# Attention scores: from two products over 128 rows per block to three products over 64 rows, two heads side by side

## The reference

```python
scores = scale * np.matmul(q, k.transpose(0, 1, 3, 2))
scores = cap * np.tanh(scores / cap)
attn = np.exp(scores - max)
attn = attn / (sum + 1e-09)
x = np.matmul(attn, v)                          # to (1792, 768)
h = np.maximum(np.maximum(x @ w1, x @ w2), x @ w3)
x = h @ w_out
silu = g * (1.0 / (1.0 + np.exp(-g)))           # g = x @ w_gate
out = (silu * (x @ w_val)) @ w_out2             # width 1536 between
```

## Time and profile before

| | |
|---|---|
| median of three runs | 1102.54 us |
| profiled execution, its own time | 1104.76 us |
| its span, first to last instruction | 1102.8 us |
| mean granted TensorE clock | 0.998 of full |
| PE busy | 1085.2 us, 98% |
| PE weight loads (PEld) busy | 980.7 us, 89% |
| DVE, ACT, POOL busy | 582.6, 475.2, 121.1 us |

### The profile page before, as it was taken

One profiled execution on the slowest core, in us unless ns is written; L12 is line 12 of the kernel. 1 busy time (PEld: TensorE's weight loads), 2 busy tenths in 40 slices (PEclk: granted clock), 3 DMA queues, 4 the chain that ended last, 5 costly groups with the idle time before them and its releaser, 6 DMA issues.

```text
span 1102.8 us, 13696 instructions
## 1 busy us (share of the span) xinstructions
PE 1085.2 (98%) x5232; PEld 980.7 (89%) x5232; DVE 582.6 (53%) x794; ACT 475.2 (43%) x601; POOL 121.1 (11%) x72
## 2 busy tenths in 40 slices
PE   6999999999999999999999999999999999999998
PEld 3669999999998999999999999999999999999998
DVE  3998777988961555557553354555664212122310
ACT  5965444444433353454452434434443322332322
POOL 0105444444340000000000000000000000000000
PEclk9999999999999999999999999999999999999999
DMA  7566763754848577577476856765555766666664
GB/s 182 121 162 219 261 211 125 265 194 144 267 148 265 180 214 210 175 213 216 171 221 224 252 177 208 220 188 197 182 172 183 234 232 208 225 210 219 218 227 134
DMA packets 98897, 222.68 MB, mean 202 GB/s; under 512 B 31249, under 2 KB 34321, under 8 KB 98833
## 3 DMA queue, kind: packets, MB, share of 16 engines
q1 hardware_dynamic: 95376, 216.31, 62.1%
q10 hardware_dynamic: 3456, 5.51, 1.3%
HBM read 192.68 MB, written 29.10 MB: 201 GB/s over the span
## 4 chain that ended last, share of the span: by engine, by line
PE 92%; ACT 3%; issue 2%; DMA 2%; SPq 0%; DVE 0%; ACTq 0%
PE moe_ps L340 78%; PE score_ps L265 6%; PE pv_ps L292 5%; PE pv_ps L297 3%; ACT prob L395 2%; DMA lo_store<-w_lo 1%; DMA qk_raw<-qk_in 1%; ACT sums L405 0%; DMA stage<-w_in 0%; ACT w_hi L386 0%; PE moe_ps L279 0%; ACT prob L398 0%; PE pv_ps L279 0%; ACT L395 0%; SPq L189 0%
## 5 line engine op out<-in xcount | busy, mean ns | idle before, releaser
L340 PE MATMUL moe_ps<-x_lo,w_hi 128*128 128x448 f32 x1008 | 369.1, 366 | 0.0
L340 PE MATMUL moe_ps<-x_hi,w_hi 128*128 128x448 f32 x1008 | 368.9, 366 | 0.0
L340 PE MATMUL moe_ps<-x_hi,w_lo 128*128 128x448 f32 x1008 | 368.5, 366 | 0.0
L386 ACT ACTIVATE w_hi<-stage 128x768 fp32r<-128x768 f32 x240 | 202.3, 843 | 341.6 <-DMA stage<-w_in 212.0
L340 PEld LDWEIGHTS moe_ps<-x_hi,w_hi 128*128 128x128 f32 x1008 | 189.7, 188 | 16.1
L340 PEld LDWEIGHTS moe_ps<-x_hi,w_lo 128*128 128x128 f32 x1008 | 189.9, 188 | 15.1
L340 PEld LDWEIGHTS moe_ps<-x_lo,w_hi 128*128 128x128 f32 x1008 | 189.9, 188 | 15.0
L340 PE MATMUL moe_ps<-gv_hi,w_hi 128*128 128x448 f32 x432 | 157.9, 365 | 0.0
L340 PE MATMUL moe_ps<-gv_lo,w_hi 128*128 128x448 f32 x432 | 157.9, 365 | 0.0
L340 PE MATMUL moe_ps<-gv_hi,w_lo 128*128 128x448 f32 x432 | 157.7, 365 | 0.0
L249 POOL TENSOR_TENSOR w_lo<-stage,w_hi 128x768 fp32r<-128x768 f32 x60 | 118.9, 1983 | 208.4 <-ACT w_hi L386 208.4
(11 more groups left out here) (50 smaller groups left out, 893.0 us busy)
## 6 DMA issues: line engine op xcount, KB each, us to landing
stage<-w_in SPq DMA_DIRECT2D x240, 384.0 KB, 4.0
w_lo<-lo_store SPq DMA_DIRECT2D x180, 384.0 KB, 3.1
lo_store<-w_lo SPq DMA_DIRECT2D x60, 384.0 KB, 3.9
qk_raw<-qk_in SPq DMA_DIRECT2D x48, 448.0 KB, 6.2
v_one<-v_in SPq DMA_DIRECT2D x48, 112.0 KB, 3.8
out<-out_sb ACTq DMA_DIRECT2D x24, 224.0 KB, 4.4
cap<-cap_in SPq DMA_DIRECT2D x1, 0.5 KB, 2.0
```

The costliest lines, as they stand in the source:

```text
L340: mm = nc.tensor.matmul(moe_ps[:, bank_of(u), 0:SEQ], w[:, u % ring, c * P:(c + 1) * P], m[:, kc, :], start=(first and c == 0 and n == 0), ...
L386: nc.scalar.activation(w_hi[:, u % R_HI, :], stage[:, u % STAGE, :], ACT.Copy).then_inc(w_hi_done, 1)
```

## The change

Each step now takes one chunk c = a % 4 of both heads. Head 0 of the pair lies on partitions 0 to 63 and head 1 on 64 to 127, for q and k alike, so that q and k are loaded once. A step has six score products over 64 rows each: for each of the three terms k_hi·q_hi, k_hi·q_lo, k_lo·q_hi one product of head 0 on the upper rows of the array and one of head 1 on the lower rows, into two different banks. The fourth term, k_lo·q_lo, is no longer made. DVE makes the high and the low part of a pair's q and k in one call of two operations, in two buffers. The sums of both heads of a pair are taken together after its last step. ACT does one tanh of a single column at the start, as soon as `cap` is loaded.

```diff
-SUMS_AT = {4: 0, 8: 1}
-PREP_AT = {3: 0, 7: 1}
+SUMS_AT = 8
+PREP_AT = 3
...
-        qk_raw = sb("qk_raw", [P, 2, 4, SEQ])
-        qk_hi = sb("qk_hi", [P, 4, SEQ], F32R)
-        q_lo = sb("q_lo", [P, 2, SEQ], F32R)
+        qk_raw = sb("qk_raw", [P, 2, 2, SEQ])
+        qk_hi = sb("qk_hi", [P, 2, 2, SEQ], F32R)
+        qk_lo = sb("qk_lo", [P, 2, 2, SEQ], F32R)
...
             def load_qk(g):
                 if g >= 2:
-                    sp.wait_ge(qk_split, 2 * (g - 1))
-                for r in range(2):
-                    sp.dma_start(qk_raw[r * HEAD_DIM:(r + 1) * HEAD_DIM, g % 2, :, :],
-                                 qk_in[g, :, :, :]).then_inc(qk_loaded[g % 2], 16)
+                    sp.wait_ge(qk_split, g - 1)
+                sp.dma_start(qk_raw[:, g % 2, :, :], qk_in[g, :, :, :]).then_inc(qk_loaded[g % 2], 16)
...
             def scores(a):
-                g, h, c = a // 4, a // 2 % 2, a % 2
-                pe.wait_ge(qk_split, 2 * g + h + 1)
+                g, c = a // 4, a % 4
+                pe.wait_ge(qk_split, g + 1)
...
-                for i in range(HALF):
-                    k0 = (HALF * c + i) * KEYS
-                    for n, q in enumerate((qk_hi[:, h, :], q_lo[:, h, :])):
-                        last = nc.tensor.matmul(score_banks(a)[0:KEYS, i, 0:SEQ],
-                                                qk_hi[:, 2 + h, k0:k0 + KEYS], q,
-                                                start=(n == 0), stop=(n == 1))
+                terms = ((qk_hi, qk_hi), (qk_hi, qk_lo), (qk_lo, qk_hi))
+                for n, (keys, queries) in enumerate(terms):
+                    for h in range(2):
+                        rows = slice(h * HEAD_DIM, (h + 1) * HEAD_DIM)
+                        last = nc.tensor.matmul(score_banks(a)[0:KEYS, h, 0:SEQ],
+                                                keys[rows, g % 2, 1, c * KEYS:(c + 1) * KEYS],
+                                                queries[rows, g % 2, 0, :],
+                                                start=(n == 0), stop=(n == 2))
...
             def take_sums(g, h):
-                act.wait_ge(value_done, 4 * g + 2 * h + 2)
+                act.wait_ge(value_done, 4 * g + 4)
...
+            act.wait_ge(cap_loaded, 16)
+            nc.scalar.activation(table_warm[:, :], cap[:, :], ACT.Tanh)
             act.wait_ge(scale_done, 2)
-            act.wait_ge(cap_loaded, 16)
             for a in range(FIRST):
                 weigh(a)
-                if a >= 2 and a % 2 == 1:
-                    take_sums((a - 2) // 4, (a - 2) // 2 % 2)
+                if a % 4 == 1 and a > 4:
+                    for h in range(2):
+                        take_sums(a // 4 - 1, h)
...
-            take_sums(PAIRS - 1, 1)
+            for h in range(2):
+                take_sums(PAIRS - 1, h)
...
-            def prepare_qk(g, h):
+            def prepare_qk(g):
                 raw = qk_raw[:, g % 2, :, :]
-                dve.wait_ge(qk_loaded[g % 2], 32 * (g // 2 + 1))
-                if g >= 1:
-                    dve.wait_ge(score_done, 4 * (g - 1) + 2 * h + 2)
-                nc.vector.tensor_copy(qk_hi[:, h::2, :], raw[:, h::2, :]).then_inc(qk_hi_done, 1)
-                dve.wait_ge(qk_hi_done, 2 * g + h + 1)
-                subtract(q_lo[:, h, :], raw[:, h, :], qk_hi[:, h, :])
-                subtract(qk_hi[low, 2 + h, :], raw[low, 2 + h, :],
-                         qk_hi[low, 2 + h, :]).then_inc(qk_split, 1)
+                dve.wait_ge(qk_loaded[g % 2], 16 * (g // 2 + 1))
+                if g >= 2:
+                    dve.wait_ge(score_done, 4 * (g - 1))
+                nc.vector.tensor_copy(qk_hi[:, g % 2, :, :], raw).then_inc(qk_hi_done, 1)
+                dve.wait_ge(qk_hi_done, g + 1)
+                subtract(qk_lo[:, g % 2, :, :], raw, qk_hi[:, g % 2, :, :]).then_inc(qk_split, 1)
...
             for g in range(PAIRS):
-                prepare_qk(g + 1, 0)
-                if g >= 1:
-                    normalise(g - 1)
-                    split_x(0, g - 1)
-                prepare_qk(g + 1, 1)
-            normalise(PAIRS - 1)
-            split_x(0, PAIRS - 1)
+                if g + 2 <= PAIRS:
+                    prepare_qk(g + 2)
+                normalise(g)
+                split_x(0, g)
```

More of the change, by code:

```diff
@@ L110, in build @@
         tanh_scale = sb("tanh_scale", [P, 1])
+        table_warm = sb("table_warm", [P, 1])
         moe_ps = ctx.enter_context(nc.psum_tensor("moe_ps", [P, BANKS, 512], F32))
@@ L158, in build @@
         sum_cols = [slice(HEAD_DIM, P), slice(0, HEAD_DIM)]
-        low = slice(HEAD_DIM, P)
         def score_banks(a):
@@ L261, in scores @@
                     pe.wait_ge(tanh_done, a - 1)
-                for i in range(HALF):
-                    k0 = (HALF * c + i) * KEYS
-                    for n, q in enumerate((qk_hi[:, h, :], q_lo[:, h, :])):
-                        last = nc.tensor.matmul(score_banks(a)[0:KEYS, i, 0:SEQ],
-                                                qk_hi[:, 2 + h, k0:k0 + KEYS], q,
-                                                start=(n == 0), stop=(n == 1))
+                terms = ((qk_hi, qk_hi), (qk_hi, qk_lo), (qk_lo, qk_hi))
[6 more added lines that the diff above has]
+                                                start=(n == 0), stop=(n == 2))
                 last.then_inc(score_done, 1)
             def values_whole(a):
-                g, h, c = a // 4, a // 2 % 2, a % 2
-                if h == 0 and c == 0:
+                g, c = a // 4, a % 4
+                if c == 0:
                     pe.wait_ge(v_loaded[g % 2], 32 * (g // 2 + 1))
@@ L276, in values_whole @@
                 pe.wait_ge(exp_done, a + 1)
[L277 to L280, removed]
+                for h in range(2):
+                    last = nc.tensor.matmul(value_banks(g)[:, h, 0:SEQ], v_one[:, g % 2, h, c, :],
+                                            prob[:, a % NP, h, :], start=(c == 0), stop=(c == CH - 1))
                 last.then_inc(value_done, 1)
             def values_split(a):
-                g, h, c = a // 4, a // 2 % 2, a % 2
-                if h == 0 and c == 0:
+                g, c = a // 4, a % 4
+                if c == 0:
                     pe.wait_ge(v_split, g - PAIRS + 1)
@@ L288, in values_split @@
                 pe.wait_ge(p_hi_done, a - FIRST + 1)
-                for i in range(HALF):
-                    j = HALF * c + i
+                for h in range(2):
                     for v in (v_hi, v_lo):
-                        nc.tensor.matmul(pv_ps[:, h, 0:SEQ], v[:, h, j, :], p_hi[:, a % NQ, i, :],
-                                         start=(j == 0 and v is v_hi), stop=False)
+                        nc.tensor.matmul(pv_ps[:, h, 0:SEQ], v[:, h, c, :], p_hi[:, a % NQ, h, :],
+                                         start=(c == 0 and v is v_hi), stop=False)
                 pe.wait_ge(p_lo_done, a - FIRST + 1)
[L295 to L298, removed]
+                for h in range(2):
+                    last = nc.tensor.matmul(pv_ps[:, h, 0:SEQ], v_hi[:, h, c, :], p_lo[:, a % NQ, h, :],
+                                            start=False, stop=(c == CH - 1))
                 last.then_inc(value_done, 1)
@@ L453, in _ @@
                     weigh(4 * g + SCORE_AT[j])
-                if g is not None and j in SUMS_AT:
-                    take_sums(g, SUMS_AT[j])
+                if g is not None and j == SUMS_AT:
+                    for h in range(2):
+                        take_sums(g, h)
             evacuate(LAST - 1)
@@ L562, in _ @@
                                     ALU.mult).then_inc(scale_done, 1)
-            for h in range(2):
-                prepare_qk(0, h)
+            prepare_qk(0)
+            prepare_qk(1)
             for g in range(PAIRS):
-                prepare_qk(g + 1, 0)
-                if g >= 1:
-                    normalise(g - 1)
-                    split_x(0, g - 1)
-                prepare_qk(g + 1, 1)
-            normalise(PAIRS - 1)
-            split_x(0, PAIRS - 1)
+                if g + 2 <= PAIRS:
+                    prepare_qk(g + 2)
+                normalise(g)
+                split_x(0, g)
             for u in range(LAST):
@@ L582, in _ @@
                         weigh(4 * g + WEIGH_AT[j])
-                    if j in PREP_AT and g + 1 < BATCH * PAIRS:
-                        prepare_qk(g + 1, PREP_AT[j])
+                    if j == PREP_AT and g + 1 < BATCH * PAIRS:
+                        prepare_qk(g + 1)
                     if j == NORM_AT:
@@ L597, in heads @@
     def heads(a):
-        return a.reshape(BATCH * PAIRS, 2, SEQ, HEAD_DIM).transpose(0, 3, 1, 2)
+        return a.reshape(BATCH * PAIRS, 2, SEQ, HEAD_DIM).transpose(0, 1, 3, 2).reshape(-1, P, 1, SEQ)
     def units(w):
```

## The result

The changed kernel has a median of 1113.72 us over four runs (1111.22 to 1115.59) beside 1102.41 us for the kernel before: a ratio of 1.010, 95% interval 1.0077 to 1.0122. It is slower by 11.3 us, where 1084 was forecast. The profiled execution took 1112.8 us with a span of 1110.9. In three of the four executions the mean granted clock was 0.998 of full (1112.80 to 1115.59 us), in the fourth it was 1.000 (1111.22). Two disturbed executions are left out of all that follows, one of the kernel before (2193.67 us) and the profiled one of e7b (1523.70 us, granted clock 0.656).

A forecast was written before the change was run, and what follows sets the result against it. PE, busy 98%, was taken as the bound, with ACT tighter in stage A. Stage B's scores -14.6 and the start -4.1 gave -18.7 us, from the median 1102.5 to 1084 us; range 1079 to 1121.

The forecast's parts named there:

- the term for the scores in stage B: Stage B, where PE is always busy: head pairs run side by side, 0.203 us less a step, -14.6 us over 72 steps.
- The sign that the prediction gave for being wrong: PE in stage B: wrong if half-row products do not overlap, or if the unit's first product waits.
- Its other estimate: Score step in stage B at 77% of ideal overlap, from the skill page: 0.79 us, term -1.2, sum about 1097 us.
- The rival: Each half/whole-row switch costs 0.16 us, +23.3 in stage B: 1108 us; dearer form 1140. Chances 0.20 to 0.2 us, 0.06 from 0.3.
- The start: Path to stage A's first tanh: load -2.5, first scores 0.37, table load 1.28 us off the path, together -4.1 us.
- Stage A: From 12.88 to 70.70 us: PE's step falls to 2.11 us, but ACT needs 2.41, so the scores gain nothing there.
- DVE, the sums, the loads: Shorter preparation on DVE, sums of both heads together, 24 fewer DMAs on SP: nothing for each.
- The long wait: Stage B at 345: PE waits 2.37 us for a tanh, then nine slow products; no term, 4 us either way.

The follow-up runs named there:

- e7b: Changed kernel with two banks for feed-forward sums, not four, and two steps' scores made per visit, 36 visits in stage B: 1095.05 us, 1097.01 when run again.
- v1: Kernel before plus 60 visits, each a pair of 64-row products with 112 weight columns, ahead of the last batch element's units: 1137.27 us, 0.582 us a visit.
- e7a: Changed kernel with two banks for feed-forward sums, not four, and a pair's last two steps moved, still one step a visit: 1109.34 us.
- e5: Changed kernel with the same products, but from the fourth unit on a step's score products split into two visits, 140 switches more: 1140.17 us.
- v3: Kernel before plus 60 visits, each a pair of 64-row products with 32 weight columns, not 112: 1132.86 us, 0.508 us a visit.
- e1: Changed kernel with four 128-row score products a step, mixing the heads, in place of the six over 64 rows: 1098.66 us, 0.9962 of before.
- e8: Changed kernel with the 64-row score products in stage A only, four full-row ones mixing the heads in stage B: 1102.67 us over ten runs.
- v4: Kernel before plus 60 visits, each a single 64-row product of the first head: 1137.23 us, 0.581 us a visit.

## Why the prediction was wrong

**The step that failed** is the term for the scores in stage B, -14.6 us, as far as it left the switches unpriced. Its first half held: two heads side by side cost what one costs, three pairs 0.61 us (0.206 for a full-row visit; the second head of a visit 0.00). But it took the cheap edges of the earlier trace rows, where all products use the whole array, for the edges of another kind. There were two switches a step at 0.188 (v1), 0.198 (e7b against e7a) and 0.189 to 0.21 us (e5). With 0.195 a step costs 0.61 + 0.39 = 1.00 us and not 0.61, against 0.81 before: +13.5 us over 72 steps in place of -14.6, and 12.5 with the 0.188 of v1, which is what the two profiled executions differ by in stage B. The sign that the prediction gave for being wrong, that the unit's first product waits, is in the rows: 0.31 us from the last pair to it. Its other estimate, 0.79 us for the six products, did not come either: the three pairs themselves go at 0.20 us each.

**The rival** had the place and the sign: a price for each switch, 1108 us, from the tail of a record at 0.16. The tail was not what set it, by v3, where 66 ns less of load took 73 ns off a visit. A nearer row stood in the earlier trace rows: the load, 0.17 to 0.19 us, which could no longer hide; that it is the whole of the price is not shown. With 0.195 for 0.16 the rival's sum gains 4.8 us in stage B and 1.7 in stage A (2.50 us a step there), 1114 us, near the 1113.7 measured. Its stage A term was right in kind and too high.

That rival had been given 0.26 of the chance in its two forms, too little for a cost that nothing in the trace excluded. What was held against it, that values and scores of stage A alternate at 0.81 + 1.50 us, excluded nothing: the 1.50 is what is left of 2.32 after the 0.81, so it would hold the price of a change of kind as well, and in stage A all products used the whole array.

The range of 1079 to 1121 takes in the measured time because it took in this rival up to 0.2 us a switch; the forecast itself was off by 30 us and had the wrong sign.

**The start**, -4.1 us, was right: the first tanh came 4.5 us earlier, of which the load 2.7 (2.5 forecast), the first scores 0.36 (0.37), DVE 0.16 (none), the table 1.3. e1 shows 3.7 to 4.4 us for all of the change but its products, of which the start is the largest part.

**Stage A** was to be hidden. PE became its pace, at 2.49 us a step, as the rival said (2.43). It costs 0.8 to 1.1 us by the starts of stage B in e8, the changed kernel and e1 (67.84, 68.12, 67.03).

**DVE, the sums, the loads** were priced at nothing; e1 bears it out, since with all of them it is faster by about the gain of the start. Its stage B begins 5.5 us earlier than before, though, and its median is 4.4 us lower at most, so up to 2 us may have been lost again in stage B; no run looks for them. **The long wait** came again, 2.6 us with nine products at half the clock behind it, inside the 4 us set for it.

The sum from the measured parts: e1's 1098.7, 13.5 for stage B and 0.8 for stage A make 1113.0, 0.7 us below the median. That it comes so near is partly luck, as the long wait, of up to 4 us, differs between executions and is in no term.

## What to carry to other kernels

Two products over 64 rows on the two halves of the array ran side by side here, loads included: the second cost nothing. But each change between half and whole of the array cost about 0.19 us, at least a part of it the weight load that is no longer hidden. So count the switches, not only the products: here a visit had to save two products (0.41 us) to pay for its two switches (0.38 to 0.40). Grouping two steps into one visit took 14 us off e7a; with the gains of the start, that made +11 us into -5 to -7. Where a trace holds no instance of a kind of change, a first guess at its price is what is hidden today only because that change never occurs; here that was a load of 0.17 to 0.19 us.

## What the runs showed that was not expected

A product over 96 rows costs what one over 128 does at its edges (0.205 against 0.206 us); of the row counts tried, only 64 paid for a switch, and it did so even with a single product (v4, 0.581 us a visit). At a switch the load path idles for 0.3 us, and the cost falls with the number of weight columns: 80 columns fewer saved 0.073 us a visit.
